# Sums of squares for the RMS norm on 64x64 tiles of the array, and an earlier store of the inverse roots

## The reference

```python
# attention: window of 64 keys, causal
scores = scale * np.matmul(q, k.transpose(0, 1, 3, 2))
scores = np.where(mask, scores, -1000000000.0)
attn = softmax(scores)                 # written out with max, exp, sum + 1e-9
x = (attn @ v) as [2304 tokens, 512]

# first MLP, with the norm
rms = np.sqrt(np.mean(x * x, axis=-1, keepdims=True) + 1e-06)
xn = x / rms * rms_g
g = xn @ w_gate                        # [512, 1536]
silu = g * (1.0 / (1.0 + np.exp(-g)))
x = silu * (xn @ w_val) @ w_out        # [1536, 512]

# second MLP
r = np.maximum(x @ w_in, 0.0)          # [512, 2048]
out = (r * r) @ w_out2                 # [2048, 512]
```

## Time and profile before

| | us |
|---|---|
| median of three runs | 869.42 (867.86 to 870.32) |
| the profiled execution, whole | 869.6 |
| its span in the profile | 867.8 |
| TensorE busy | 851.2 (98%) |
| VectorE busy | 588.8 (68%) |
| ScalarE busy | 477.2 (55%) |
| GpSimd busy | 468.0 (54%) |
| HBM traffic | 80.5 MB read, 19.4 MB written |

### The profile page before, as it was taken

The page is one execution under the profiler, slowest core; times in us unless marked ns, Lnnn a source line. Parts: engine busy times, 40 slices in busy tenths (PEclk is TensorE's granted clock), DMA queues, the critical chain, the costliest instruction groups (busy, mean ns, idle before and its releaser), DMA issues.

```text
span 867.8 us, 16812 instructions
## 1 busy us (share of the span) xinstructions
PE 851.2 (98%) x6390; PEld 839.5 (97%) x6390; DVE 588.8 (68%) x729; ACT 477.2 (55%) x1001; POOL 468.0 (54%) x471
## 2 busy tenths in 40 slices
PE   7898999999999999999999999999999999999998
PEld 6787999999999999999999999999999999999998
DVE  4668776468557558755557767678677777677982
ACT  6787566545565645555554455554455454555451
POOL 4656398493589665388857368222187212386100
PEclk9999999999999999999999999999999999999999
DMA  8773122322222232222222322256622266523587
GB/s 300 246 225 88 49 74 74 64 77 61 82 72 73 74 73 61 79 74 74 73 56 61 85 68 74 55 164 225 218 86 71 71 222 185 169 73 98 179 254 246
DMA packets 109871, 100.98 MB, mean 116 GB/s; under 512 B 8544, under 2 KB 87520, under 8 KB 109792
## 3 DMA queue, kind: packets, MB, share of 16 engines
q1 hardware_dynamic: 92544, 84.04, 32.8%
q10 hardware_dynamic: 17248, 15.87, 5.5%
HBM read 80.48 MB, written 19.40 MB: 115 GB/s over the span
## 4 chain that ended last, share of the span: by engine, by line
PE 91%; DVE 3%; issue 2%; ACT 2%; POOL 1%; DVEq 0%; POOLq 0%; ACTq 0%
PE banks L840 29%; PE banks L841 29%; PE banks L842 29%; ACT probs L1165 1%; PE banks L810 1%; DVE probsT L1498 1%; PE banks L751 1%; PE banks L824 1%; PE banks L784 1%; DVE acts L1438 0%; DVE banks L1478 0%; PE banks L759 0%; POOL h L689 0%; POOL d_lo L696 0%; DVE xc_lo L1629 0%
## 5 line engine op out<-in xcount | busy, mean ns | idle before, releaser
L840 PE MATMUL banks<-xc_hi,w_hi 128*128 128x384 f32 x844 | 282.5, 335 | 0.2 <-DVE xc_lo L1470 0.2
L842 PE MATMUL banks<-xc_hi,w_lo 128*128 128x384 f32 x844 | 281.9, 334 | 0.0
L841 PE MATMUL banks<-xc_lo,w_hi 128*128 128x384 f32 x844 | 281.9, 334 | 0.0
L840 PE MATMUL banks<-hs_hi,d_hi 128*128 128x384 f32 x544 | 182.3, 335 | 0.8 <-POOL d_lo L696 0.6
L842 PE MATMUL banks<-hs_hi,d_lo 128*128 128x384 f32 x544 | 181.7, 334 | 0.0
L841 PE MATMUL banks<-hs_lo,d_hi 128*128 128x384 f32 x544 | 181.7, 334 | 0.0
L840 PEld LDWEIGHTS banks<-xc_hi,w_hi 128*128 128x128 f32 x844 | 158.4, 188 | 0.6 <-DVE xc_lo L1470 0.4
L841 PEld LDWEIGHTS banks<-xc_lo,w_hi 128*128 128x128 f32 x844 | 158.4, 188 | 0.0
L842 PEld LDWEIGHTS banks<-xc_hi,w_lo 128*128 128x128 f32 x844 | 158.4, 188 | 0.0
L1414 DVE TENSOR_TENSOR w_lo<-w_raw,w_hi 128x1024 fp32r<-128x1024 f32 x58 | 75.6, 1303 | 82.1 <-ACT w_hi L1086 81.8
L578 POOL TENSOR_TENSOR w_raw<-w_raw 128x256 f32<-128x256 f32 x58 | 61.8, 1065 | 122.1 <-DVE d_lo L1584 52.2
(11 more groups left out here) (115 smaller groups left out, 1333.7 us busy)
## 6 DMA issues: line engine op xcount, KB each, us to landing
w_kept<-stash SPq DMA_DIRECT2D x56, 256.0 KB, 3.2
w_raw<-in_w_gate SPq DMA_DIRECT2D x36, 256.0 KB, 2.9
w_raw<-in_w_val SPq DMA_DIRECT2D x72, 128.0 KB, 2.9
d_raw<-in_w_out SPq DMA_DIRECT2D x36, 256.0 KB, 2.6
d_raw<-in_w_down SPq DMA_DIRECT2D x32, 256.0 KB, 2.9
v_sb<-in_v_rows SPq DMA_DIRECT2D x16, 384.0 KB, 4.3
w_raw<-in_w_in SPq DMA_DIRECT2D x24, 256.0 KB, 2.7
w_raw<-in_w_in SPq DMA_DIRECT2D x48, 128.0 KB, 2.6
```

The costliest lines, as they stand in the source:

```text
L840: pe.matmul(ps, w_h, v_h, start=first, stop=False, skip_group_check=joined)
L841: pe.matmul(ps, w_h, v_l, start=False, stop=False, skip_group_check=joined)
L842: return pe.matmul(ps, w_l, v_h, start=False, stop=last, skip_group_check=joined)
```

## The change

Four parts.

1. `token_sums` splits each of its six matmuls into four on 64x64 tiles: for each half a of the partitions that are summed over and each half b of the tokens of a block. The sums of the two halves a go to two banks.
2. `first_sums` is split likewise, but in two calls for each batch c: `first_sums(c, 0)` over the lower half of the partitions and `first_sums(c, 1)` over the upper one. Both write to bank 5, in columns of their own, WIDE = 32 wide. The call with a = 0 now stands inside the slot (10 or 12), after the scores and, in slot 10, ahead of the value product, in slot 12 after it and ahead of the transposes; the call with a = 1 stands where the whole batch stood. A new semaphore, part_summed, keeps the halves apart.
3. VectorE's `mean_square` first adds the two halves (a reduction over an innermost axis of two, into rms), waits for that (ms_joined), and then scales in place.
4. ScalarE issues `rinv_store` in step 9 instead of step 10.

```diff
-WIDE = 64
+WIDE = 32
...
+                if g == 10:
+                    pe.wait_ge(consts, CONSTS)
+                    pe.wait_ge(sq_pool, KT)
+                    first_sums(0, 0)
                 if 0 <= g - PV_LAG < GROUPS:
                     value_product(g - PV_LAG)
+                if g == 12:
+                    pe.wait_ge(sq_pool, KT + 2)
+                    pe.wait_ge(sq_done, 2)
+                    first_sums(1, 0)
...
-            def token_sums(q, ps):
+            def token_sums(q, banks):
 
                 pe.wait_ge(sq_sum, 3 * q)
                 for n in range(TB):
-                    mm = pe.matmul(ps[:, n:n + 1], sq_total[:, n * P:(n + 1) * P], ones[:, 0:1],
-                                   start=True, stop=True)
+                    for a, b in ((0, 0), (1, 1), (0, 1), (1, 0)):
+                        to = n * P + b * WIN
+                        mm = pe.matmul(banks[a][rows(b), n:n + 1], sq_total[rows(a), to:to + WIN], ones[rows(a), 0:1],
+                                       start=True, stop=True)
                 mm.then_inc(ms_mm, 1)
 
-            def first_sums(c, ps):
-
+            def first_sums(c, a):
+
+                if (c, a) != (0, 0):
+                    pe.wait_ge(part_summed, 2 * c + a)
                 for n in range(c * TB // 2, (c + 1) * TB // 2):
+                    at = (a * TB + n) * WIDE
                     for k in range(KT):
-                        mm = pe.matmul(ps[:, n * WIDE:(n + 1) * WIDE], squares[0][k][:, n * P:(n + 1) * P], ones[:, 0:WIDE],
-                                       start=k == 0, stop=k == KT - 1)
-                if c == 1:
-                    mm.then_inc(ms_mm, 1)
+                        for b in range(2):
+                            to = n * P + b * WIN
+                            mm = pe.matmul(bank[5][rows(b), at:at + WIDE], squares[0][k][rows(a), to:to + WIN],
+                                           ones[rows(a), 0:WIDE], start=k == 0, stop=k == KT - 1)
+                mm.then_inc(ms_mm if (c, a) == (1, 1) else part_summed, 1)
...
-                if g == 10:
-                    pe.wait_ge(consts, CONSTS)
-                    pe.wait_ge(sq_pool, KT)
-                    first_sums(0, bank[5])
-                if g == 12:
-                    pe.wait_ge(sq_pool, KT + 2)
-                    pe.wait_ge(sq_done, 2)
-                    first_sums(1, bank[5])
+                if g in (10, 12):
+                    first_sums((g - 10) // 2, 1)
...
-                        token_sums(r + 1, v_banks(r)[0])
+                        token_sums(r + 1, v_banks(r)[0:2])
...
-                        if s == 10:
+                        if s == 9:
                             rinv_store(r + 1)
...
-                of = ps[:, 0:TB] if q else ps[:, 0:TB * WIDE].rearrange("p (n w) -> p n w", n=TB)[:, :, 0]
-                nc.vector.tensor_scalar(rms[:], of, 1.0 / D, 1e-6, ALU.mult, ALU.add).then_inc(ms_done, 1)
+                nc.vector.tensor_reduce(rms[:], parts, AX_X, ALU.add).then_inc(ms_joined, 1)
+                dve.wait_ge(ms_joined, q + 1)
+                nc.vector.tensor_scalar(rms[:], rms[:], 1.0 / D, 1e-6, ALU.mult, ALU.add).then_inc(ms_done, 1)
```

More of the change, by code:

```diff
@@ L278, in build @@
         sq_done, sq_sum, ms_mm, ms_done = sem("sq_done"), sem("sq_sum"), sem("ms_mm"), sem("ms_done")
+        part_summed, ms_joined = sem("part_summed"), sem("ms_joined")
         rms_done, rinv_done, diag_done = sem("rms_done"), sem("rinv_done"), sem("diag_done")
@@ L1424, in low2, with mean_square @@
                                         ALU.subtract).then_inc(lo2_done, 1)
-            def mean_square(q, ps):
+            def mean_square(q, parts):
                 dve.wait_ge(ms_mm, q + 1)
-                of = ps[:, 0:TB] if q else ps[:, 0:TB * WIDE].rearrange("p (n w) -> p n w", n=TB)[:, :, 0]
-                nc.vector.tensor_scalar(rms[:], of, 1.0 / D, 1e-6, ALU.mult, ALU.add).then_inc(ms_done, 1)
+                nc.vector.tensor_reduce(rms[:], parts, AX_X, ALU.add).then_inc(ms_joined, 1)
+                dve.wait_ge(ms_joined, q + 1)
+                nc.vector.tensor_scalar(rms[:], rms[:], 1.0 / D, 1e-6, ALU.mult, ALU.add).then_inc(ms_done, 1)
             def inverse(q):
@@ L1503, in _ @@
                 if g == 12:
-                    mean_square(0, bank[5])
+                    sums_of = bank[5][:, 0:2 * TB * WIDE].rearrange("p (a n w) -> p a n w", a=2, n=TB)
+                    mean_square(0, sums_of[:, :, :, 0].rearrange("p a n -> p n a"))
                 if g == 13:
@@ L1652, in _ @@
                     if s == 8 and r + 1 < PAIRS:
-                        mean_square(r + 1, v_banks(r)[0])
+                        mean_square(r + 1, banks2[2 * ((r + 1) % 2)][:].rearrange("p (a c) -> p c a", a=2)[:, 0:TB, :])
                     if s == 9 and r + 1 < PAIRS:
```

## The result

The changed kernel takes 876.42 us (872.99 to 878.67, 8 runs) against 869.43 us (867.86 to 870.68, 8 runs) before: ratio 1.0077, 95% interval 1.0063 to 1.0091. That is 7.3 us above the forecast of 869.1 and outside the range. The profiled execution took 876.86 us with a span of 875.1.

What follows compares the result with a forecast made beforehand. TensorE was taken to hold 91% of the chain of waits, which passes through both batches of sums of squares. First sums +1.8, token sums -0.6 and store -1.6 gave -0.4 us: 869.42 to 869.1 us, range 866.5 to 871.7.

Steps and rivals of the forecast that it cites:

- The rate of the tiled sums: First sums on 64x64 tiles in one row half: 29.3 ns a record, 1.41 us for each call of 48 records.
- rivals 1 to 3: First-sum calls take 0.64 us (865.9 in all, 11%), 2.8 us (874.6, 6%) or 2.04 us (871.5, 8%).
- The token sums: Later layers' sums, two places: an insertion costs 1.06 us instead of 1.34, gain 0.28 us each, -0.6 us together.
- The store: Inverse roots stored one step sooner: ScalarE's wait for the landing and TensorE's gap in the first pair go, -1.6 us.
- rival 4: The store's move does nothing for TensorE, as the landing slips too or d_lo is late otherwise: 870.7 us, 10%.
- the second pair gives nothing: Second pair of token tiles: the earlier store brings no gain there.
- The term of group 10: First half call ahead of value product 7 waits for GpSimd's squares: scores of group 11 at 47.29 instead of 46.18, +1.1 us.
- the +1.8 for groups 10 and 12: Attention part: both moved batches of first sums delay the scores of group 13 by 1.8 us in all, kept whole.
- rival 5: Granted clock falls to half in the longer waits of groups 10 to 12, costing up to 1.7 us: 870.8, 10%.
- the 0.7 more that the forecast had for group 12: Second batch of first sums: delay grows from +1.1 us at group 11 to +1.8 at group 13.

Runs made afterwards that it cites:

- e6: e3 with SyncE's loads of K, Q and V for sequence block 12 held until the first half call is done: ratio 1.0091.
- e4: Kernel before with whole-array first sums, each whole batch moved to the new places (ahead of value product 7 and the transposes of group 10): ratio 1.0074.
- f3: Changed kernel plus full-array matmuls with unused results ahead of the waits of groups 10 and 12 and of each second half call: ratio 1.0051.
- e5: e3 with both tiled half calls together at the old place, behind the transposes: ratio 1.0061.
- e7: Kernel before with WIDE = 32 instead of 64 in the whole-array first sums, nothing else: ratio 1.0024.
- f1: Kernel before with WIDE = 1 instead of 64 in the whole-array first sums: ratio 1.0029.
- e1: Kernel before with only the store of the inverse roots moved from step 10 to 9: 868.50 us against 871.81, ratio 0.9962.
- f4: Kernel before with the store in step 9 and WIDE = 85 instead of 64 in the first sums: 869.12 us, ratio 0.9982.
- e3: Kernel before with only the first sums changed (tiled halves, moved calls), store and token sums as before: 879.73 us, ratio 1.0091.

## Why the prediction was wrong

**What was right.** The rate of the tiled sums (1.37 us a call, forecast 1.41), which rules out rivals 1 to 3: no call took 0.64, 2.8 or 2.04 us. The last of these was the rule of the Trainium skill's page "TensorE: Matmul & The Clock Gate" (Part 3, "The mechanism") on weight loads within a row group; the trace does not agree with it here, 29 ns a record instead of the 43 that load and stream in turn would give. The token sums were right as well (-0.33 by the insertion's 1.34 and 1.01, forecast -0.28). The store helped as described, which rules out rival 4, but that its term came out at 1.6 between two traces was luck: the trace of before is the shortest of nine behind T1, the others and the runs say about 3, and "the second pair gives nothing" does not hold in e6, where TensorE waits 0.8 us for `sbb` and `d_lo` there too.

**The term of group 10.** Forecast +1.1, of it 1.0 of wait. I took the end of GpSimd's squares, 42.62, from one execution as if it stood still. It ended at 43.63 in the change, and TensorE waited 1.42 us. Without any late half clock the two moved waits cost 2.7 us in e4, not 1.8. The mechanism was right, the term was 0.9 too small: the value product and the transposes had covered not only the mean wait but its scatter too.

**The step that failed** is the +1.8 for groups 10 and 12 as the whole delay, with everything else on TensorE's side left to rival 5: "With waits of 1.2 us at most between busy batches, 10%", at a price of up to 1.7 us. Two things were wrong in it. The clock at half was not a one-in-ten case, and the silences, idle time without a semaphore, were put at nothing.

*The clock.* It fell in five of the six profiled kernels with tiled first sums (all but f3), for 6.8 or 10.2 us, and for 6.8 in both with fewer columns. In the change itself the fall at 49.57 follows 3.41 us with only 1.30 busy, the silence among them, much like the fall in the earlier trace rows; so there idling would do as the reason, only it was longer than the 1.2 us that I had allowed. But in e5, e7 and f1 the clock fell without any moved wait. I asked only how long TensorE would stand idle, and looked at two rows that differ in that. The experiments show that the kind of work matters as well: whole-array sums of 64 columns held the clock in every trace at the old places, and tiles of 64x64 with 32 columns, or whole-array sums with 32 columns or one, mostly did not (f3 apart), though in e5 (but for two breaks of 0.3 us), e7 and f1 the engine was issuing all through the sums. I had counted the columns as free because they don't change the pace, about 110 ns for 64 and for one. They are free in the sums and not in what follows. The Trainium skill's page "TensorE: Matmul & The Clock Gate" (Part 1) ties the clock to how busy the engine has been and gives waits as the example; f1's fall after 3.41 busy us of 3.41 is a case that busy time as the profile counts it does not explain. Which quantity does is not settled here.

*The silences.* The change has one of 2.3 us in the second call, and two more in its chain behind the first sums, 0.95 and 1.25 us. These end 1.3 and 1.5 us after the next 16,384 bytes have landed (at 63.46 and 68.39; TensorE goes on at 64.76 and 69.84):

```profile
63.81 0.95 issue
...
68.59 1.25 issue
```

Before has five such silences, the longest from 25.08 to 27.10, inside the first window of the earlier trace rows; I had read that window for the clock alone. All five lie ahead of the first sums, of the change's seven four lie in or behind them.

**The sum, mended**, by the delays of the score groups. At group 11, +4.6: the forecast's 1.1, squares that end 0.7 later from S0 than forecast, the silence with 2.3 and the half clock in the second call with 0.5. At group 12, +7.2: between the two groups TensorE works almost all through at half clock, 5.15 us for what took 2.59. At group 13, +6.7: the 0.7 more that the forecast had for group 12 did not come. By group 15, +9.3: the two later silences, 2.2 us, lie in between. So the miss of 7.2 us in S0 to T1 (9.05 instead of 1.8) is made of about 3 us of half clock, 4.5 us of silences and 0.7 of squares, less about 1 that other waits took back. This is the account of one execution.

**The same from the runs.** One level for each kernel and one slope in the mean clock, fitted to all 170 runs, gives 0.56 us (standard error 0.05) for each 0.001 of clock. The change's mean clock of 0.9930 is 0.0056 below the 0.9986 that before has in the other sets, so 3.1 of the 7.0 us between the medians go with the clock; 3.9 remain, against a forecast of -0.4. How large this rest is depends on the runs of before: those of the later sets, 2 us slower, would leave 1.3, and no run here says why the sets differ. The slope is a mean clock's; 0.001 of it are 1.7 us at half clock, so it gives 0.3 us for each, as e7's trace does (2.2 for 6.83). Taken back to full clock in this way, e4 is 3.2 us above the before of its set, e7 and f1 0.5 and 0.1, and e5 3.7 (standard errors 0.5 to 0.7). So columns alone cost by the clock only, places cost in both ways, and so do tiles at the old places, of which the longer sums explain about 1 us; the rest is open.

Whether the clock falls in a given run varies (e4: 0.986 to 0.998), so the profiled executions show kinds of loss rather than their mean. T1 to T2 and T2 to the end also scatter in the kernels that keep the store in step 10: 140.1 to 141.9 and 588.6 to 591.3 us, against 138.7 and 588.6 to 588.8 in e1 and f4; these are the waits shown under e1.

## What to carry to other kernels

Before moving a wait ahead of work that covers it, take the spread of its releaser over several executions, not its time in one; the cover pays for the late ones. Before making TensorE's small work smaller (fewer columns, quarter tiles) in a part that is bound by other engines, ask what the granted clock will do in the microseconds behind it: where records cost the same with 64 columns as with one, the 64 may be worth keeping. Read a gain from more than one trace where there are several: the store's move was worth 1.6 us against one trace and 3 against nine. And take a change apart: here a store moved by one step gave 0.38% (0.24 to 0.52), and the rest of the change took more than that back.

## What the runs showed of the hardware

- TensorE's granted clock halved directly behind stretches that the profile counts as 95 to 100% busy, when these held 64x64 tiles with 32 columns (e5) or full-array matmuls of one column (f1).
- Matmul records of 64x64 tiles with 32 columns in one row half: 48 start within 1.37 us, 29 ns each; over all four tiles with one column: 48 in 0.88 us, 18 ns each, the drain included. Full-array records at full clock: 108 to 113 ns with 1, 32, 64 and 85 columns alike.
- In all 14 traces TensorE stands still at the end of some blocks of 256 of its records, and each of these silences (0.3 to 2.9 us between two starts) ends 1.2 to 1.6 us after the next 16,384 bytes have landed. The Trainium skill's page "Runtime: NRT & Kernel Launch" ("Instruction fetch mechanics") calls the crossing of such a boundary "mostly hidden"; before and e1 show it hidden at this place, the change and e3 do not.
- GpSimd's squares begin at 41.01 in before and at 41.73 in e1, whose program is the same up to there.
